# First expert's weight split dealt out by columns at the end of attention; the parts of the first pair of heads copied by ScalarE, with turns of the identity in TensorE's early gaps

## What is computed

```python
mask = q_bucket[:, :, :, None] == k_bucket[:, :, None, :]
scores = np.where(mask, scale * np.matmul(q, k.transpose(0, 1, 3, 2)), -1000000000.0)
attn = np.exp(scores - np.max(scores, axis=-1, keepdims=True))
attn = attn / (np.sum(attn, axis=-1, keepdims=True) + 1e-09)
x = np.matmul(attn, v)                      # then laid out as tokens x 512
...
for e in range(E):                          # first mixture, dense
    out += P[:, e:e + 1] * (np.maximum(x @ w1[e], 0.0) @ w2[e])
...
for e in range(E):                          # second mixture, one expert per token
    out[mask] = gate_w[mask, None] * (np.maximum(x[mask] @ w1[e], 0.0) @ w2[e])
```

## Time and profile before

| | |
|---|---|
| median of 3 runs | 1600.26 us (1598.87 to 1602.89) |
| the profiled execution's own time | 1600.57 us |
| its span, first to last instruction | 1598.5 us |
| PE, PEld busy | 1569.7 us (98%), 1308.4 us (82%) |
| DVE, ACT, POOL busy | 685.9 us (43%), 507.9 us (32%), 333.3 us (21%) |
| mean granted TensorE clock | 0.992 |
| PE's share of the chain that ended last | 96% |

### The profile page before, as it was taken

One profiled execution on the slowest core, in us unless ns is written; L12 is line 12 of the kernel. 1 busy time (PEld: TensorE's weight loads), 2 busy tenths in 40 slices (PEclk: granted clock), 3 DMA queues, 4 the chain that ended last, 5 costly groups with the idle time before them and its releaser, 6 DMA issues.

```text
span 1598.5 us, 21713 instructions
## 1 busy us (share of the span) xinstructions
PE 1569.7 (98%) x7539; PEld 1308.4 (82%) x7540; DVE 685.9 (43%) x1235; ACT 507.9 (32%) x933; POOL 333.3 (21%) x563
## 2 busy tenths in 40 slices
PE   8999998999999999999999999999999999999997
PEld 7999997778888888888888888888888887788886
DVE  6888886342211211222221121122222255787666
ACT  4887885112100101211210011021121133576554
POOL 4565556100300210030030021003004000222222
PEclk9999999999999999999999999999999999899999
DMA  6645662100110110110020011011002121674310
GB/s 156 149 111 133 151 167 78 53 1 0 53 54 1 53 52 0 52 52 0 0 105 0 0 52 52 0 52 52 0 0 105 40 73 73 216 277 152 133 46 25
DMA packets 45415, 110.75 MB, mean 69 GB/s; under 512 B 5814, under 2 KB 7862, under 8 KB 45376
## 3 DMA queue, kind: packets, MB, share of 16 engines
q1 hardware_dynamic: 41488, 101.11, 20.4%
q0 software_dynamic: 3424, 8.14, 1.5%
q10 hardware_dynamic: 464, 0.98, 0.3%
HBM read 81.57 MB, written 8.13 MB: 56 GB/s over the span
## 4 chain that ended last, share of the span: by engine, by line
PE 96%; DVE 1%; issue 1%; ACT 1%; SPq 0%; POOL 0%; DMA 0%; DVEq 0%; POOLq 0%; ACTq 0%
PE psum L463 26%; PE psum L465 26%; PE psum L464 26%; PE psum L743 4%; PE psum L732 2%; PE psum L756 2%; PE psum L757 2%; PE psum L733 2%; PE psum L714 1%; PE psum L1069 1%; PE psum L770 1%; PE psum L878 1%; PE psum L1060 0%; PE psum L872 0%; PE psum L801 0%
## 5 line engine op out<-in xcount | busy, mean ns | idle before, releaser
L1239 ACT ACTIVATE h_hi<-psum 128x512 fp32r<-128x512 f32 x192 | 114.7, 598 | 897.8 <-PE psum L465 897.8
L463 PE MATMUL psum<-xt_lo,w_hi 128*128 128x512 f32 x768 | 306.6, 399 | 4.4 <-issue 4.4
L465 PE MATMUL psum<-xt_hi,w_lo 128*128 128x512 f32 x768 | 305.3, 397 | 0.0
L464 PE MATMUL psum<-xt_hi,w_hi 128*128 128x512 f32 x768 | 305.1, 397 | 0.0
L463 PE MATMUL psum<-w_lo,h_hi 128*128 128x512 f32 x768 | 302.1, 393 | 0.0
L465 PE MATMUL psum<-w_hi,h_lo 128*128 128x512 f32 x768 | 299.2, 390 | 0.0
L464 PE MATMUL psum<-w_hi,h_hi 128*128 128x512 f32 x768 | 299.1, 389 | 0.0
L1661 DVE SCALAR_TENSOR_TENSOR h_lo<-psum,h_hi 128x512 fp32r<-128x512 f32 x192 | 132.7, 691 | 373.2 <-ACT h_hi L1239 373.1
L494 POOL CAST w_hi<-w_raw 128x512 fp32r<-128x512 f32 x68 | 42.6, 627 | 814.5 <-PE psum L465 814.3
L1724 DVE SCALAR_TENSOR_TENSOR tok<-psum,route,tok 128x512 f32<-128x512 f32 x83 | 56.8, 744 | 354.6 <-PE psum L465 354.6
L463 PEld LDWEIGHTS psum<-xt_lo,w_hi 128*128 128x128 f32 x768 | 145.1, 189 | 39.7 <-issue 4.6
(11 more groups left out here) (279 smaller groups left out, 2021.4 us busy)
## 6 DMA issues: line engine op xcount, KB each, us to landing
w_raw<-in_moe_w_dram SPq DMA_DIRECT2D x25, 2048.0 KB, 8.2
w_raw_odd<-in_moe_w_dram SPq DMA_DIRECT2D x4, 2048.0 KB, 10.3
k_hh<-k_hi SPq DMA_DIRECT2D x32, 192.0 KB, 3.0
w_raw_even<-in_moe_w_dram SPq DMA_DIRECT2D x3, 2048.0 KB
x_rows<-tok SPq DMA_DIRECT2D x14, 256.0 KB, 2.5
k_raw<-in_k_dram SPq DMA_DIRECT2D x8, 384.0 KB, 3.2
v_raw<-in_v_dram SPq DMA_DIRECT2D x16, 192.0 KB, 3.4
k_b<-k_lo SPq DMA_DIRECT2D x16, 192.0 KB, 3.4
```

The lines of the kernel that those rows point to most:

```text
L463: pe.matmul(acc, a[0], b[1], start=start, stop=False)
L464: pe.matmul(acc, a[0], b[0], start=False, stop=False)
L465: return pe.matmul(acc, a[1], b[0], start=False, stop=stop)
L1239: act.activation(h_s[0][:, f, :], psum[:, f % 4, :], ACT.Relu).then_inc(m1.h_hi, 1)
```

## The change

At the start:

- SP's queue loads k ahead of `proj`, ACT's queue q ahead of `proj`. ScalarE first takes one exponential of one column (into a buffer that is overwritten later), which brings its table load there.
- The hi and lo parts of `proj` share a tile, so that 16 placements become 8 of twice the columns; four for k, then the cast of q, then four for q. VectorE clears two tiles instead of four.
- Three DMAs of ACT's queue and one of SP's (`q_t[0]` twice, `q_b[0]`, `k_b[0]`) become four ScalarE copies of 64x768.
- TensorE turns the identity 5 times ahead of the constants' matmuls and 20 times behind them (14 before), and 12 times between tiles 1 and 2. Tile 2 goes to banks 6 and 7 and does not wait for an exponential.
- VectorE writes the bits of k's second half ahead of q's; tiles 0 to 2 need only q's first half, and tile 3 waits for the other on a semaphore of its own. The bits for head 1 come behind the row minima of tiles 0 and 1.
- SP loads the second pair ahead of the moves for head 1, and those no longer wait for head 0's.

At the hand-over: for every kd, ScalarE and VectorE split columns 0 to 511, GpSimd columns 512 to 1023. ScalarE's cast of kd = 0 stands behind step G-2, VectorE's subtraction behind step G-1; GpSimd's kd = 0 stands behind step G, kd = 1 to 3 behind the last tile of attention output. f = 0 waits for the first halves, f = 4 for the second.

```diff
@@ SP
+        sp.dma_start(k_raw[:], k[0]).then_inc(s_k_in, 16)
         sp.dma_start(proj_raw[0:D, :], proj).then_inc(s_proj_in, 16)
-        sp.dma_start(k_raw[:], k[0]).then_inc(s_k_in, 16)
...
-        sp.wait_ge(s_qk_split, 1)
-        sp.wait_ge(s_zeroed, 2)
-        move_part(sp, k_b[0][0:D, :], k_lo, s_k_moved[0])
-        sp.wait_ge(s_k_moved[0], 64)
-        sp.wait_ge(s_q_moved[0], 64)
+        load_pair(1)
         sp.wait_ge(s_zeroed, 4)
-        move_k(sp, 1)
+        move_k(sp, 1, s_first_moved)
...
-        load_pair(1)
@@ GpSimd
+        def first_w1(kd):
+            a = slice(512, FF)
+            pool.wait_ge(s_sc, G)
+            pool.wait_ge(m1.w1_in, 16)
             copy(w1_s[0][:, kd, a], w1_raw[:, kd, a]).then_inc(s_first_cast, 1)
...
+        def beside_last(g):
+            if g == G:
+                first_w1(0)
+        run_steps(pool, step, after=beside_last)
         outputs(NH // 2 - 1, 1, 1)
+        for kd in range(1, KD):
+            first_w1(kd)
@@ TensorE
+        def turn_identity(times, bank):
+            for i in range(times):
+                pe.transpose(psum[:, bank, 0:P], ident[:], ident[:])
+        pe.wait_ge(s_ident, 1)
+        turn_identity(5, 0)
         pe.wait_ge(s_const, 1)
...
+        turn_identity(20, 1)
...
         scores(0, 0, 1, first=True)
-        scores(0, 0, 2)
-        pe.wait_ge(s_bits, 2)
+        turn_identity(12, 7)
+        scores(0, 0, 2, first=True)
...
-                            pe.wait_ge(*((s_first_lo, kd) if 0 < kd < KD - 1 else (s_first_pool, 4 if kd else 2)))
+                            pe.wait_ge(s_first_lo, kd + 1)
                             pe.wait_ge(m1.xt_lo, kd + 1)
+                        if first and c == 0 and f == KF // 2:
+                            pe.wait_ge(s_first_pool, kd + 1)
@@ ScalarE
+        act.wait_ge(s_ident, 1)
+        act.activation(prob[0][:, 0, 0:1], ident[:, 0:1], ACT.Exp)
...
-        move_part(act, q_t[0][0:D, :], q_hi, s_q_moved[0])
-        move_part(act, q_b[0][0:D, :], q_hi, s_q_moved[0])
+        place_part(q_t[0][0:D, :], q_hi, s_q_moved[0])
+        place_part(q_b[0][0:D, :], q_hi, s_q_moved[0])
+        act.wait_ge(s_qk_split, 1)
+        place_part(k_b[0][0:D, :], k_lo, s_k_moved[0])
         act.wait_ge(s_qk_split, 2)
-        move_part(act, q_t[0][D:P, :], q_lo, s_q_moved[0])
+        place_part(q_t[0][D:P, :], q_lo, s_q_moved[0])
...
-            act.copy(w1_s[0][:, kd, :], w1_raw[:, kd, :]).then_inc(s_first_hi, 1)
+            act.copy(w1_s[0][:, kd, 0:512], w1_raw[:, kd, 0:512]).then_inc(s_first_hi, 1)
...
+            if g == G - 2:
+                first_w1_hi(0)
             if g == G:
                 x_t_hi(m1, 0, 2, 2)
-                first_w1_hi(1)
-                first_w1_hi(2)
+                for kd in range(1, KD):
+                    first_w1_hi(kd)
@@ VectorE
+        first_bits(0, slice(0, 32), q_b[0]).then_inc(s_q_moved[0], 16)
+        first_bits(0, slice(HK, HK + 32), k_b[0])
+        dve.wait_ge(s_proj, 2)
+        first_bits(1, slice(HK, HK + 32), k_b[0]).then_inc(s_k_moved[0], 16)
+        first_bits(1, slice(0, 32), q_b[0]).then_inc(s_q_bits, 1)
+        row_terms(0, 0, 0)
+        row_terms(0, 0, 1)
         for half in range(2):
             hash_bits(half, 0, bank=4 + half)
...
+            if g == G - 1:
+                first_w1_lo(0)
             if g == G + 1:
-                first_w1_lo(1)
-                first_w1_lo(2)
+                for kd in range(1, KD):
+                    first_w1_lo(kd)
```

More of the change, by code:

```diff
@@ L165, in program @@
     proj_raw = place("proj_raw", [P, BITS], F32, beside[5])
-    proj_s = [place(f"proj_{part}", [P, BITS], F32R, beside[5]) for part in ("hi", "lo")]
-    proj_w = [[place(f"proj_{s}_{part}", [P, P], F32R, at) for part in ("hi", "lo")] for s in "qk"]
-    proj_mix = place("proj_k_mix", [P, P], F32R, at)
+    proj_s = place("proj_parts", [P, 2, BITS], F32R, beside[5])
+    proj_w = [place(f"proj_{s}", [P, 2, P], F32R, at) for s in "qk"]
     consts_row = place("consts_row", [1, 2 * P], F32, beside[5])
@@ L277, in at_first, with score_bank @@
         return isinstance(g, int) and g == 0
+    def score_bank(g, t):
+        return 6 if isinstance(g, int) and g == 2 else 2 * (t % 2)
     def preparation(it, kk):
@@ L499, in split_qk @@
             if r == -1:
-                for u in range(2):
-                    pool.wait_ge(s_k_moved[u], 64 * i)
+                pool.wait_ge(s_k_moved[0], 64 * i)
+                if isinstance(i, int) and i == 1:
+                    pool.wait_ge(s_first_moved, 48)
+                    pool.sem_inc(s_k_moved[1], 48)
+                else:
+                    pool.wait_ge(s_k_moved[1], 64 * i)
                 pool.wait_ge(s_k_in, 16 * i + 16)
@@ L688, in _ @@
         mm.then_inc(s_const_t, 1)
-        pe.wait_ge(s_ident, 1)
-        for i in range(14):
-            pe.transpose(psum[:, i % 4, 0:P], ident[:], ident[:])
+        turn_identity(20, 1)
         pe.wait_ge(s_ident, 2)
@@ L700, in hash_pair @@
                 if first:
-                    pe.wait_ge(s_k_proj, 8)
+                    pe.wait_ge(s_k_proj, 4)
             else:
@@ L713, in hash_pair @@
                     for src in parts:
-                        mm = pe.matmul(psum[:, bank, 0:HALF], w[part][:], src[:, a],
+                        mm = pe.matmul(psum[:, bank, 0:HALF], w[:, part, :], src[:, a],
                                        start=(w is proj_w[1] and part == 1 and src is k_lo),
@@ L727, in scores @@
                 pe.wait_ge(s_q_moved[u], 64 * it + 64)
+            if isinstance(g, int) and g == 3:
+                pe.wait_ge(s_q_bits, 1)
             a = slice(t * P, t * P + P)
             for c in range(2):
-                o = psum[:, 2 * (t % 2) + c, 0:HALF]
+                o = psum[:, score_bank(g, t) + c, 0:HALF]
                 b = slice(c * HALF, (c + 1) * HALF)
@@ L737, in turn_probs @@
             for c in range(2):
-                if not at_first(g):
+                if at_first(g):
+                    pe.wait_ge(s_bits, c + 1)
+                else:
                     pe.wait_ge((s_lo_a, s_lo_b)[c], g)
@@ L805, in _ @@
             hash_pair(0, half, 4 + half)
-        for i in range(8):
-            pe.transpose(psum[:, i % 4, 0:P], ident[:], ident[:])
+        turn_identity(8, 0)
         scores(0, 0, 0, first=True)
         scores(0, 0, 1, first=True)
-        scores(0, 0, 2)
-        pe.wait_ge(s_bits, 2)
+        turn_identity(12, 7)
+        scores(0, 0, 2, first=True)
         def beside_last(g):
@@ L1155, in _, with place_part @@
                 for c, sign in ((u * D + at_bits, -1.0), (u * D + at_bits + BITS, 1.0)):
-                    for w, part in zip(w_parts, proj_s):
-                        act.activation(w[rows, c:c + BITS], part[rows, :].bitcast(F32), ACT.Copy,
-                                       scale=sign).then_inc(placed, 1)
+                    act.activation(w[rows, :, c:c + BITS], proj_s[rows, :, :].bitcast(F32), ACT.Copy,
+                                   scale=sign).then_inc(placed, 1)
+        def place_part(dst, src, moved):
+            act.copy(dst, src[0:D, :].bitcast(F32)).then_inc(moved, 16)
+        act.wait_ge(s_proj_split, 2)
+        act.wait_ge(s_proj_zeroed, 1)
+        place_projection(proj_w[1], HK, s_k_proj)
         act.wait_ge(s_q_in, 16)
         act.activation(q_hi[:], q_raw[:], ACT.Copy, scale=-SCALE).then_inc(s_qk_hi, 1)
+        place_projection(proj_w[0], 0, s_q_proj)
         act.wait_ge(s_qk_hi, 2)
         act.wait_ge(s_zeroed, 2)
-        move_part(act, q_t[0][0:D, :], q_hi, s_q_moved[0])
-        move_part(act, q_b[0][0:D, :], q_hi, s_q_moved[0])
+        place_part(q_t[0][0:D, :], q_hi, s_q_moved[0])
+        place_part(q_b[0][0:D, :], q_hi, s_q_moved[0])
+        act.wait_ge(s_qk_split, 1)
+        place_part(k_b[0][0:D, :], k_lo, s_k_moved[0])
         act.wait_ge(s_qk_split, 2)
-        move_part(act, q_t[0][D:P, :], q_lo, s_q_moved[0])
+        place_part(q_t[0][D:P, :], q_lo, s_q_moved[0])
         exp(0, 0, 0)
@@ L1348, in _ @@
         for w in proj_w:
-            for part in range(2):
-                link(dve.memset(w[part][:].bitcast(F32), 0.0))
+            link(dve.memset(w[:].rearrange("p a b -> p (a b)").bitcast(F32), 0.0))
         dve.sem_inc(s_proj_zeroed, 1)
```

56 lines of the change are left out of this document (25 added, 31 removed).

## The result

| | before | changed |
|---|---|---|
| median | 1600.66 us (1598.87 to 1602.89, 4 runs) | 1589.14 us (1588.11 to 1589.57, 4 runs) |
| profiled execution: time, span | 1600.57, 1598.5 us | 1588.11, 1586.1 us |
| mean granted TensorE clock | 0.992 | 0.996 |

What follows compares the result with a forecast made beforehand. TensorE, busy 98% of the span, was taken as the bound, so only its gaps and slow stretches could be won. 3.1 + 1.9 + 6.5 = 11.5 us gave 1589.1, stated as 1589.0 us; range 1586 to 1594.

Steps and rivals of the forecast that it cites:

- A: Kernel start until the first score, 14.45 us before: 3.1 us won, between 0.6 and 4.1.
- B: From the first score to head 1's, 14.0 us before: 1.9 us won, between 0.9 and 2.4.
- C: Hand-over from attention to the mixture: 6.5 us won, the 4.43 us gap and 2.07 of slow stretch; 5.7 with longer subtractions.
- Rival 1: Start: the clock stays low until the hash is done; A = 0.6, B = 1.6, 1591.9 us; chance 0.2.
- the two items: First score to head 1's: tile 2 not waiting for tile 0's exponential, 0.9 us; earlier second-pair load, 0.97 us.
- Rival 2: Hand-over keeps a wait, from VectorE meeting GpSimd's pair or kd = 0 pushing turned probabilities: 1591.0 us at most; chance 0.12.
- Rivals 3 and 4: 3: start's gain taken back, 1594.1 us, chance 0.08; 4: GpSimd becomes the bound behind the hand-over, 1593.7, chance 0.02.

Runs made afterwards that it cites:

- experiment 1: The two halves apart: the hand-over part put into the kernel before, 1592.91 us; the changed kernel with before's hand-over, 1596.19 us.
- The changed kernel again: The changed kernel itself, nothing altered, timed once more beside two kernels that load `proj` first: 1588.85 us, ratio 0.9931 to before.
- the run of the hand-over alone: The kernel before with only the hand-over part of the change, its old start kept: 1592.91 us, ratio 0.9956.
- experiment 5: The changed kernel with GpSimd's three pairs (kd = 1 to 3) ahead of the last tile of attention output instead of behind it: 1593.71 us.

## Why the prediction was right, and where its steps were not

The forecast was 1589.0 us, the median is 1589.14. The sum of 11.5 us agrees, and that is luck in part: A was forecast 1.25 us too large, B 0.46 too small. By the marks the lead is 11.17 us in this pair of profiles, and 10.4 to 11.3 by the two halves of experiment 1.

- **A, forecast 3.1 us, measured 1.85.** First score at 12.60 instead of 11.35, in three parts. *Operands*, 0.55 us, which is all but 0.02 of what they were to win: `proj` landed behind k and q as I took it, but its split took 0.92 us and not 0.5 (5.28 to 6.20), k's placements 0.65 and not 0.5, so q_lo ended at 8.75 and not 8.2. *Clock and turns*, 0.6 us: I had the clock up by 7 or 8 us and gave a late rise a chance of 0.2. It rose at 9.4; the 20 turns, which I charged for only in that case, kept the k part waiting until 7.97, so that it ended at half speed at 9.40, 0.6 behind q's operands. The changed kernel again settles these two: there the clock was up as forecast, and the first score came at 12.01, with q_lo still at 8.75. *The rest*, 0.1 us, is the bits. Rival 1 in full, A = 0.6, did not happen: 12 matmuls took 2.2 us, not 4.1. But that the 2.0 us of the clock are the turns' doing is not shown. In the run of the hand-over alone the old start had its clock up by 8.9 us as well, and its first score came at 13.04. With the clock early in both, the start wins 1.0 us at the first score (13.04 to 12.01), with it late in both 1.85, and across the draws 0.4 to 2.4.
- **B, forecast 1.9 us, measured 2.36**, the upper bound of 2.4 with "some of the half-speed stretch". Tile 2 measured 0.62 to 0.86 us of the 0.9. The load I had priced by GpSimd's wait, 0.97, as if the two items simply added. GpSimd's cast of k starts when both its row terms are done and k is there. In before the row terms ended 9.17 us behind the first score and the wait for k 10.14; now the row terms end at 7.82, and k is there. So the row terms gained 1.35 us where tile 2 was to give 0.9, and only the early load let that count: put back late in the changed kernel it makes the cast start at 10.10 again, loses 2.32 of the 2.36 us up to head 1 and, with the slow stretch behind, costs 4.1. "What is late next is the GpSimd work itself" held: ScalarE waits 0.82 us for the row bias at 23.11. The lead is still 4.12 us at 58 us; another 0.4 came from there to the last turn, in small pieces that I have not placed.
- **C, forecast 6.5 us, measured 6.66.** f = 0 took 2.88 us for 2.80, subtractions of 0.62 each for 0.67, no wait at kd = 3. Rival 2 did not come, and experiment 5 shows what keeps it out: GpSimd's order, with the attention output ahead of the three pairs.
- **ScalarE's copies.** "The DMAs that they replace would land 2.2 to 4.3 us after issue, which is no slower" failed: 6.0 to 6.7 us for the fourth. In before the three of ACT's queue did land 3.3, 3.8 and 4.1 us after issue; in the new order head 1's moves and a fourth one are beside them. It did not touch the sum, which was built on the copies' own 0.83 us; they ended at 11.48, 1.1 us ahead of the first score.
- **Rivals 3 and 4.** No sign of either: nothing of the start's lead was taken back up to M, and the w2 splits ended at 281.9 us, ahead of the first matmul on w2 at 291.74.

The difference of the two profiled spans, 12.4 us, is 1.2 more than the lead at M; it arises behind M, within the 2 us by which that stretch scatters. The medians differ by 11.5.

## What to carry to other kernels

Measure a change at marks behind each of its parts, not by the total: here the stretch behind the change scatters by 2 us, while the stretch from first score to M repeats within 0.15. Price a gap of TensorE with the half-speed stretch that can follow: it cost half of the gap or more (1.7 us behind 2 to 3 us of waits, 2.07 behind 4.43), or nothing. When two causes end at one wait, find out which ends last before adding them: undoing the load alone took back all that both had brought up to head 1. And price a transfer from rows with the same company in the queues: four 192 KB moves in a row took 2.6 us for the first and 6.7 for the last, where ScalarE's copy took 0.83 each.
